# Softmax of an attention front end: exp head by head on ScalarE with its row sum, copies of q and k ahead of it, and loads in another order

## The reference, cut to what matters

```python
def sm_attn(qq, kk, vv):                      # B=2, H=8, D=64
    s = scale * np.matmul(qq, kk.transpose(0, 1, 3, 2))
    s = s - np.max(s, axis=-1, keepdims=True)
    a = np.exp(s)
    a = a / (np.sum(a, axis=-1, keepdims=True) + 1e-09)
    return np.matmul(a, vv)
# 1. S=576 positions, averaged by 4 (Sd=144): full attention, result repeated 4 times ("down")
out_up = np.repeat(sm_attn(q_d, k_d, v_d), 4, axis=2)
# 2. local attention on the full positions: |i - j| < 4, all else -1e9 before the softmax
out_local = ...softmax(where(mask, scale * q @ k.T, -1e9)) @ v
x = out_up + out_local                        # 1152 tokens x 512
# 3. top-1 routing to 8 experts, relu(x w1) w2 (512 -> 1024 -> 512), times the gate
# 4. (h * tanh(softplus(h))) @ w_out with h = x @ w_in (512 -> 2048 -> 512)
```

## Time and profile before

| | us |
|---|---|
| median of the runs | 500.51 |
| the profiled execution, its own time | 498.48 |
| its span, first to last instruction | 496.7 |
| PE busy | 457.3 (92%) |
| VectorE busy | 289.4 (58%) |
| ScalarE busy | 218.7 (44%) |
| GpSimd busy | 127.0 (26%) |

### The profile page before, as it was taken

One profiled execution on the slowest core, in us unless ns is written; L12 is line 12 of the kernel. 1 busy time (PEld: TensorE's weight loads), 2 busy tenths in 40 slices (PEclk: granted clock), 3 DMA queues, 4 the chain that ended last, 5 costly groups with the idle time before them and its releaser, 6 DMA issues.

```text
span 496.7 us, 10187 instructions
## 1 busy us (share of the span) xinstructions
PE 457.3 (92%) x3580; PEld 422.6 (85%) x3581; DVE 289.4 (58%) x675; ACT 218.7 (44%) x467; POOL 127.0 (26%) x121
## 2 busy tenths in 40 slices
PE   8674869997789999999999999999999999999993
PEld 8574759886789999999999889999999999999982
DVE  4975555798910110110101179988888888888883
ACT  2454432354032332332223456655665555655541
POOL 8050271412100000000000456533353333353202
PEclk9986996999899999999999999999999999999999
DMA  9999992421357998898676422331231212141001
GB/s 187 185 174 169 223 334 86 168 93 50 114 191 251 326 324 315 273 356 284 216 286 200 155 75 46 83 75 52 58 134 47 80 42 86 42 149 42 0 1 63
DMA packets 72005, 74.94 MB, mean 151 GB/s; under 512 B 32800, under 2 KB 47776, under 8 KB 71968
## 3 DMA queue, kind: packets, MB, share of 16 engines
q1 hardware_dynamic: 70240, 69.71, 48.3%
q0 software_dynamic: 1728, 4.72, 2.5%
HBM read 64.98 MB, written 9.44 MB: 150 GB/s over the span
## 4 chain that ended last, share of the span: by engine, by line
PE 76%; DVE 12%; issue 3%; DMA 2%; ACT 2%; POOL 2%; SPq 1%; another core or an unknown queue 0%; POOLq 0%; ACTq 0%; DVEq 0%
PE ps L1074 73%; DVE mx L860 2%; DVE pr L864 1%; PE ps L1288 1%; DMA qk_tok<-in_q 1%; DMA xg<-x_by_expert 1%; PE ps L1145 1%; DVE sm L870 1%; DMA x_by_expert<-x_sb,xslot 1%; DVE qdT L831 1%; ACT kT L623 1%; POOL vd L542 1%; POOL vd L539 1%; POOL v4s L540 0%; DVE kdT L831 0%
## 5 line engine op out<-in xcount | busy, mean ns | idle before, releaser
L574 POOL TENSOR_TENSOR wiL<-raw,wiH 128x512 fp32r<-128x512 f32 x48 | 61.9, 1290 | 257.0 <-ACT wiH L623 153.6
L1074 PE MATMUL ps<-xe,raw 128*128 128x128 f32 (+2 forms) x512 | 70.0, 298 | 1.5 <-issue 0.9
L1074 PE MATMUL ps<-hid,raw 128*128 128x128 f32 (+2 forms) x512 | 70.9, 297 | 0.6 <-ACT hid L732 0.6
L1074 PEld LDWEIGHTS ps<-xe,raw 128*128 128x128 f32 x512 | 68.7, 191 | 2.3 <-issue 1.4
L1074 PEld LDWEIGHTS ps<-hid,raw 128*128 128x128 f32 x512 | 69.0, 191 | 0.8 <-issue 0.8
L1074 PE MATMUL ps<-x2L,wiH 128*128 128x384 f32 x192 | 65.3, 340 | 0.0
L1074 PE MATMUL ps<-x2H,wiH 128*128 128x384 f32 x192 | 65.1, 339 | 0.2 <-DVE x2L L990 0.2
L1074 PE MATMUL ps<-x2H,wiL 128*128 128x384 f32 x192 | 64.7, 337 | 0.0
L1074 PE MATMUL ps<-woH,gH 128*128 (+1 forms) x144 | 56.9, 395 | 1.9 <-DVE gL L990 1.9
L990 DVE TENSOR_TENSOR woL<-wo_in,woH 128x1024 f32 x8 | 9.8, 1225 | 83.3 <-ACT woH L623 83.3
L1074 PE MATMUL ps<-woH,gL 128*128 (+1 forms) x144 | 57.2, 397 | 0.0
(11 more groups left out here) (130 smaller groups left out, 752.6 us busy)
## 6 DMA issues: line engine op xcount, KB each, us to landing
raw<-in_moe_w SPq DMA_DIRECT2D x32, 1024.0 KB, 5.7
raw<-in_moe_w_in SPq DMA_DIRECT2D x24, 512.0 KB
x_by_expert<-x_sb SPq DMA_DIRECT2D x1, 4608.0 KB, 16.3
xg<-x_by_expert SPq DMA_DIRECT2D x8, 512.0 KB, 3.6
wo_in<-in_moe_w_out SPq DMA_DIRECT2D x8, 512.0 KB, 7.8
v<-in_v SPq DMA_DIRECT2D x4, 576.0 KB
qk_tok<-in_k SPq DMA_DIRECT2D x8, 256.0 KB, 5.0
qk_tok<-in_q SPq DMA_DIRECT2D x8, 256.0 KB, 5.1
```

The lines of the kernel that those rows point to most:

```text
L574: nc.gpsimd.tensor_tensor(wiL[:, r, :, :], raw_wi_tile(r), wiH[:, r, :, :].bitcast(F32), ALU.subtract).then_inc(s_wil, 1)
L1074: return T.matmul(out_, a, b, start=start, stop=stop, skip_group_check=True)
```

## The change

The constant NEG is no longer divided by SCALE, and q is scaled as ScalarE copies it. VectorE's subtraction (L864) and row sum (L870) are gone: VectorE gives the negated maximum (for down steps in two instructions), and ScalarE computes exp straight from PSUM, one instruction for each head (8 for a local step, 4 for a down step) with the maximum as its per-row bias and the row sum as its second output. On ScalarE the copies of k and q come ahead of `exps(n)`. On VectorE the two reads of the router's counts come ahead of the maximum. PE waits for exp where it waited for the subtraction, since exp now reads the scores' banks. SP's order of loads changes. PE's last expert goes into the loop, with a branch around the transposes for the next one.

```diff
-            for t in range(6, 8):
+            for t in range(6, NT):
                 load_qk(t)
+            load_v4(2)
+            load_v4(3)
             sp.dma_start(wg...)
             for g in range(BPB):
                 load_vwin(g)
-            load_qk(8)
-            load_v4(2)
-            load_v4(3)
             for g in range(BPB, NB):
                 load_vwin(g)
...
             def exps(n):
-                kind = STEPS[n][0]
-                act.wait_ge(s_sub, n + 1)
-                if kind == "down":
...
-                    nc.scalar.activation(a, a, ACT.Exp, scale=SCALE).then_inc(s_exp, 1)
+                down = STEPS[n][0] == "down"
+                rows, nh, w = (QROWS[STEPS[n][2]], 2, SD) if down else (P, 4, WIN)
+                act.wait_ge(s_mx, n + 1)
+                if n >= 2:
+                    act.wait_ge(s_pt, n - 1)
+                for a in range(2):
+                    for h in range(nh):
+                        i = a * nh + h
+                        last = nc.scalar.activation(
+                            pr[0:rows, n % 2, a, h * w:(h + 1) * w], ps[0:rows, 2 * (n % 2) + a, h * w:(h + 1) * w], ACT.Exp,
+                            bias=mx[0:rows, n % 2, i:i + 1], scale=1.0 / FACTOR ** 2 if down else 1.0,
+                            accum_out=sm[0:rows, n % 2, i:i + 1])
+                last.then_inc(s_exp, 1)
...
-                if n < NS:
-                    exps(n)
                 if turned(n) is not None:
                     k_copy(turned(n))
                     q_copy(turned(n))
+                if n < NS:
+                    exps(n)
...
-            def stats(n):
+            def stats(n, counted):
                 dve.wait_ge(s_sc, n + 1)
-                V.tensor_reduce(st(mx), sc, X, ALU.max).then_inc(s_mx, 1)
-                dve.wait_ge(s_mx, n + 1)
-                if n >= 2:
-                    dve.wait_ge(s_pt, n - 1)
-                V.tensor_tensor(pb, sc, st(mx)..., ALU.subtract).then_inc(s_sub, 1)
+                if counted is not None:
+                    read_counts(counted)
+                if STEPS[n][0] == "down":
+                    V.tensor_reduce(st(sme), sc, X, ALU.max).then_inc(s_mxd, 1)
+                    dve.wait_ge(s_mxd, sum(is_down(m) for m in range(n + 1)))
+                    V.tensor_scalar(st(mx), st(sme), -1.0 / FACTOR ** 2, None, ALU.mult).then_inc(s_mx, 1)
+                else:
+                    V.tensor_reduce(st(mx), sc, X, ALU.max, negate=True).then_inc(s_mx, 1)
...
                 dve.wait_ge(s_exp, n + 1)
-                V.tensor_reduce(st(sm), pb, X, ALU.add).then_inc(s_sum, 1)
-                dve.wait_ge(s_sum, n + 1)
...
-                        pe.wait_ge(s_sub, n - 1)
+                        pe.wait_ge(s_exp, n - 1)
...
-            with pe.Fori(0, E - 1) as e:
-                expert(e, False)
-            expert(E - 1, True)
+            with pe.Fori(0, E) as e:
+                expert(e)
```

More of the change, by code:

```diff
@@ L27 @@
 SCALE = 1.0 / float(np.sqrt(D))
-NEG = -1.0e9 / SCALE
+NEG = -1.0e9
 EPS = 1e-9
@@ L245, in build @@
         s_tq, s_tk, s_qTc, s_kTc, s_qd = sem("q_transposed"), sem("k_transposed"), sem("qT_ready"), sem("kT_ready"), sem("qkd_ready")
-        s_sc, s_mx, s_sub, s_exp = sem("scores"), sem("row_max"), sem("scores_less_max"), sem("probs")
-        s_sum, s_den, s_rec, s_nrm = sem("row_sum"), sem("row_den"), sem("row_recip"), sem("probs_normed")
+        s_sc, s_mx, s_mxd, s_exp = sem("scores"), sem("row_max_negated"), sem("pooled_row_max"), sem("probs_and_sums")
+        s_den, s_rec, s_nrm = sem("row_den"), sem("row_recip"), sem("probs_normed")
         s_pt, s_ptc, s_av, s_avc = sem("probsT"), sem("probsT_copied"), sem("attn_out"), sem("attn_out_copied")
@@ L626, in q_copy @@
                 act.wait_ge(s_tq, t + 1)
-                copy(qT[:, :, t * P:(t + 1) * P], ps[:, qk_banks(t)[0], :].rearrange("p (h t) -> p h t", h=HP)
-                     ).then_inc(s_qTc, 1)
+                nc.scalar.activation(qT[:, :, t * P:(t + 1) * P], ps[:, qk_banks(t)[0], :].rearrange("p (h t) -> p h t", h=HP),
+                                     ACT.Copy, scale=SCALE).then_inc(s_qTc, 1)
             def k_copy(t):
@@ L923, in route, with read_counts @@
                 V.tensor_tensor(cum[:, t + 1, :], cum[:, t, :], oh[:, t, :], ALU.add).then_inc(s_cum, 1)
-            def place(t):
-                c = slice(t, t + 1)
+            def read_counts(t):
                 dve.wait_ge(s_cnt, t + 1)
@@ L932, in place @@
                 V.tensor_scalar(cmin[:, t, :], counts, float(CAP), None, ALU.min).then_inc(s_rc, 1)
+            def place(t):
+                c = slice(t, t + 1)
                 dve.wait_ge(s_rc, 2 * t + 2)
@@ L954, in _ @@
                 if n < NS:
-                    stats(n)
+                    stats(n, count_turn(n))
                 if count_turn(n) is not None:
+                    if n >= NS:
+                        read_counts(count_turn(n))
                     place(count_turn(n))
@@ L1221, in counts @@
                 if n >= NS:
-                    pe.wait_ge(s_sub, NS)
+                    pe.wait_ge(s_exp, NS)
                 if t >= 2:
@@ L1298, in transpose_rest, with expert @@
                 pe.wait_ge(s_x3c, e + 1)
-            def expert(e, last):
+            def expert(e):
                 count = tokens_of(pe, e)
@@ L1306, in expert @@
                     by_width(pe, count, lambda w: result(e, half, w))
-                    if half == 0 and not last:
-                        pe.wait_ge(s_hr, (e + 1) * M1)
-                        transpose_x(e + 1)
+                    if half == 0:
+                        with pe.If(e < E - 1):
+                            pe.wait_ge(s_hr, (e + 1) * M1)
+                            transpose_x(e + 1)
             def hidden(e, half, w):
```

1 line of the change is left out of this document (removed).

## The result

| | before | after |
|---|---|---|
| median of the runs, us | 500.0 (498.82 to 500.56, 4 runs) | 486.98 (485.81 to 487.34, 4 runs) |
| ratio, 95% interval | | 0.9739 [0.9712, 0.9765] |
| the profiled execution, its own time, us | 498.48 | 487.26 |
| its span, us | 496.7 | 484.8 |

Some executions fall into a slower state with a lower granted clock; only one run did here, at 483.4 us, of the kernel with the sums first and exp whole in all steps, and it is left out.

What follows compares the result with a forecast made beforehand. Attention was taken as one chain through PE, ScalarE and GpSimd with three long PE holes, VectorE pacing late rounds. Gains 11.2 early plus 2.7 late, 13.9 us, from 500.5 gave 486.6; likeliest range 484 to 489, 8 in 10 from 480 to 495.5.

Steps and rivals of the forecast that it cites:

- The price of a head: ScalarE's exp with sum, one head of 70 columns: 0.33 us, bounds 0.11 to 0.53; local step 2.65, down step 1.55.
- The early part, ScalarE's queue: ScalarE busy without a break from round 1 on; tile 7's q copied at 39.3 us, not 45.6, gaining 6.3.
- The step that failed: PE's hole before the first `attend` shrinks from 5.04 to about 2.3 us, and the clock stays up there.
- the chain that I summed: From tile 7's copied q to tile 8's: 4.7 us at full clock plus two copies, 0.95, ending at 44.9.
- the early gain: Up to `attend` of step 7, which was to start at about 61.3 us and not 72.48: 11.2 us gained.
- The placing and the sums: GpSimd places from 51.1, last sum of v 10.1 us later; PE's hole stays 3.1 to 4.1 us, clock falls.
- The rival with the clock up there: Clock stays up behind the hole before `attend` of step 7: 4.4 us more, 482.2 us; chance 0.17.
- The middle and the late rounds: Nothing gained from 83.81 to about 97; late rounds gain 2.7 us as PE, not VectorE, sets the pace.
- step 14's two instructions: VectorE's two long instructions gone, counted once in the round of step 14: 1.43 us, the least late gain.
- What I cost at nothing: Load order, extra VectorE instruction, counts' reads, q's scale put at no gain; expert loop's branch 0, within +0.5 and -0.5.
- v's local rows: Batch 0's in at 48 to 50 us, wanted at 54; the rival that they come late: 488.6 us, chance 0.06.

Runs made afterwards that it cites:

- the sums first and exp whole in all steps: Change with GpSimd's third and fourth sum of v ahead of its placing, and exp one instruction a step, subtraction and row sum on VectorE: 478.79 us, ratio 0.9569.
- first hole filled: Change plus 32 warm-up matmuls in PE's 2.75 us hole ahead of the first `attend`: 491.44 us, ratio 0.9818.
- the sums first: Change with GpSimd's third and fourth sum of v ahead of its placing of steps 3 to 5: 479.72 us, ratio 0.9614.
- the last hole filled: Change plus 40 warm-up matmuls in PE's 3.19 us hole ahead of `attend` of step 7: 490.55 us, ratio 0.9819.
- copies-only kernel: Kernel before with one edit, ScalarE's copies of k and q ahead of exp: 487.38 us, ratio 0.9768.
- filled, same length: Change plus 32 matmuls in the hole before the first `attend`, filling run behind the last counts cut from 90 to 58 matmuls: 482.68 us, ratio 0.9688.
- sums first, exp whole early: Change with GpSimd's third and fourth sum of v ahead of placing, exp one instruction in the first ten steps, by head after: 478.32 us, ratio 0.9553.
- sums first, old loads: Change with GpSimd's third and fourth sum of v ahead of placing, and the old order of loads: 486.47 us, ratio 0.9731.
- the longer program: Change with the filling run behind the last counts made 122 matmuls of 118 columns, not 90 of 160, no hole filled: 492.71 us, ratio 0.9856.

## Why the prediction was right, and where it was wrong

**The price of a head.** I took 0.33 us; measured 0.29, and 2.35 us a local step against 2.65; a down step 30.89 to 32.33 = 1.44 against 1.55. Both lie inside the bounds. The sum isn't free: its readout adds 0.09 us between starts. The record of an ACTIVATE with 70 columns is 335 ns, mean of 72. By the rule of the Trainium skill ("ScalarE: Activation LUTs", What ACT_TABLE_LOAD costs), 280 ns and 0.833 ns a column, it would be 338 (an estimate), and the trace agrees. With the Trainium skill's overlap of 93 ns the next instruction would start 0.245 us behind it (an estimate too); in the trace the readout starts 0.20 us behind (14.12 to 14.32).

**The early part, ScalarE's queue.** Tile 7's q was to be copied at 39.3; it was at 40.0 (39.40 and its record). Exp was cheaper than I had put it, which gave some time back, and a wait of 1.02 us at 29.65 took more: it is for PE, which ran slow (the 16 warm-ups at 25.71 took 1.66 us, not 1.27) behind a hole of 2.31 us. I had said that ScalarE has no break.

**The step that failed: "At that length I expect the clock to stay up, as at 56.01."** The hole came out at 2.75 us instead of 2.3, and the granted clock fell: 2.79 us for the 16 matmuls. From the first `attend` to the second it took 8.97 us where I had 5.6. With the hole filled it was 5.78, so the chain that I summed was right and the clock was the error of this stretch, 3.2 us. It carried through, with the 0.8 us by which the first `attend` came later than 39.3: `attend` of step 7 at 65.17, not 61.3, so the early gain was 7.3 us and not 11.2. A hole of the forecast length would not have been safe either: with the sums first it was 2.33 us, and the clock up to the second `attend` was 0.77 (7.41 us). The one hole of before with the clock up, 2.46 us, was too little to rest the step on, and I should have given it two ends.

**The placing and the sums.** Placing to last sum 10.1 us, as predicted (54.94 to 65.03), and the hole of 3.19 lies in the range that I gave. The clock fell there, as I let it. The rival with the clock up there was priced at 4.4 us, and the kernel with the sums first bears the price out: 6.63 us from `attend` of step 7 to the next instead of 10.86, so 4.2. Filling the hole gave 2.7 of it, at a clock of 0.79.

**The middle and the late rounds.** 2.7 us predicted, 2.8 measured (55.02 to 52.22). Again the size is right and the reading only in part, and some of the size is chance: the change's trace has one local round of 6.36 us where all the others with exp by head have 5.57. The 1.43 us of step 14's two instructions came out as 1.44 in the stretch from the last scores to the last counts. But VectorE's 6.08 us didn't set the pace of all local rounds: in the copies-only kernel VectorE keeps it, and PE's scores still come every 5.57. The slower rounds of the trace before followed 1.94 us in which VectorE itself was idle, with a releaser that the profile can't name, and this varies from one execution to the next: the change has such a stall of 2.66 us in VectorE, the other kernels with exp by head have none. Exp by head is worth 1.1 us in the late part by the copies-only kernel and 0.6 by the two with the sums first.

**What I cost at nothing.** Loads and loop: 0 in the median, as said. No `attend` of a local tile waited for v's local rows (the first, at 57.81, has no hole before it); how much cover they had I didn't measure.

**What made the number right.** Early 3.9 us short. On the other side: 1.0 us between the last counts and the experts, where PE waited 1.90 for DMA before and not at all in the change's trace; 0.76 in the experts; and 0.1 in the late part. That leaves the span 11.9 us shorter, and the profiled execution's own time 11.2, not 13.9. The medians are 13.0 us apart, since that execution of the change lies 0.3 us above its median and that of before 1.5 below its own. So gains that I had not forecast, and scatter, hid an early part that was 3.9 us short, 3.2 of it the failed step. That the number came out was luck.

## What to carry to other kernels

Put what other engines wait for ahead of what they don't, on each engine's queue: in this kernel moving two copies ahead of exp was worth 12 us, while taking 1.5 us of VectorE's work off each step was worth nothing that could be measured, as PE's own work set the pace of most late rounds. Before speeding up what stands ahead of a wait, look at how long PE will then stand at it: here PE came 2.1 us earlier to the same wait and lost 2.4 us by the clock. And when matmuls are added as a filler, keep the length of the program ahead of a loop as it was, or measure the loop again: 32 matmuls more cost 6 us somewhere else.

## What the runs showed of the hardware

- Exp with its row sum is an ACTIVATE (335 ns for 128x70) and a readout (220 ns, mean of 80), and the pair takes 0.29 us start to start; for 96x144 it is 0.36 us.
- The hole of PE before the first `attend`, and what came behind it:

| kernel | hole, us | the 16 matmuls, us | to the second `attend`, us | granted clock up to it |
|---|---|---|---|---|
| first hole filled | 0.29 | 1.54 | 5.78 | 1.00 |
| filled, same length | 0.54 | 1.54 | 5.97 | 1.00 |
| copies only | 0.93 | 1.54 | 6.32 | 1.00 |
| sums first, exp whole | 1.05 | 1.54 | 7.32 | 0.77 |
| sums first, exp whole early | 1.58 | 1.54 | 7.37 | 0.77 |
| sums first | 2.33 | 1.80 | 7.41 | 0.77 |
| sums first, old loads | 2.79 | 1.54 | 7.38 | 0.77 |
| the change, old loop | 2.79 | 2.79 | 8.64 | 0.65 |
| the change | 2.75 | 2.79 | 8.97 | 0.62 |

The change with the old loads (2.74), the longer program (2.82) and the last hole filled (2.88) took 8.94 to 8.98 us. So the 16 matmuls alone don't tell whether the clock fell: behind the 2.79 us hole with the sums first they took 1.54 us, and the 12 warm-ups two microseconds later 1.50, where they take 0.99 with the first hole filled.

```profile
39.43 1.54 PE L1084 MATMUL ps<-vd,prT 72*96 72x64 f32 x16 [2.79 <-issue]
...
41.47 1.50 PE L1084 MATMUL ps<-warmb 128*128 128x160 bf16 x12
```

Nor does the length of the hole settle it alone: two holes of 2.79 us ended in 7.38 and 8.64 us. The Trainium skill ("TensorE: Matmul & The Clock Gate", Part 1: The HAM clock gate) says that the chip judges activity in a window that runs on its own and doesn't start with the kernel. By that, equal holes can end either way, and these two agree.
- PE's program, 32 matmuls longer with the same number of columns, lengthened the stretch of the experts by 6.0 us, all in its first pass (a stop of 3.56 us at the first branch, 0.65 with the length restored; one of 1.31 us with nothing to wait for; and most of the rest at a lower clock). With 40 matmuls more, the stop inside the run of equal matmuls came 7 matmuls earlier.
